# Capped attention and two feed-forward layers on one core: early products moved, the slots' banks joined two slots sooner, the last store halved

## What is computed

```
q, k, v: (2, 12, 448, 64); cap = 30
scores = cap * tanh(q @ k.T / sqrt(64) / cap)
attn   = exp(scores - max(scores));  attn /= sum(attn) + 1e-9
x      = (attn @ v) as (896, 768)
h = x @ w_in (768, 2048);   g = where(h > 0, h, exp(min(h, 0)) - 1);  x = g @ w_out
h = x @ w_in2;              g = max(0.01 h, h);                        y = g @ w_out2
```

## Time and profile before

| | us |
|---|---|
| median of 3 runs | 569.2 |
| lowest and highest | 568.25 and 569.87 |
| the profiled execution's own time | 569.0 |
| its span, first to last instruction | 567.2 |
| TensorE's granted clock | 1.00 of full speed, throughout |

### The profile page before, as it was taken

How to read it: one execution, slowest core, us unless ns; L and a number is a source line. 1 busy time by engine, 2 the same in 40 slices (tenths; PEclk the granted TensorE clock), 3 DMA queues, 4 the chain that set the end, 5 groups by cost and what they waited for, 6 DMA issues and landing times.

```text
span 567.2 us, 8613 instructions
## 1 busy us (share of the span) xinstructions
PE 555.2 (98%) x2908; PEld 500.5 (88%) x2908; DVE 469.7 (83%) x760; ACT 350.3 (62%) x603; POOL 285.7 (50%) x277
## 2 busy tenths in 40 slices
PE   6999999999999999999999999999999999999997
PEld 5777789899998999999999999999999998999996
DVE  5899998998785134898989999989999789999871
ACT  6999998989995445654644455536454445544440
POOL 6779999699966655552000008967576520000000
PEclk9999999999999999999999999999999999999999
DMA  5466655645333233335644422031123226436241
GB/s 173 105 157 150 148 150 134 153 114 140 95 88 76 83 112 111 112 110 166 210 135 159 139 87 82 1 112 57 58 63 103 62 80 226 143 110 218 85 173 50
DMA packets 34172, 67.07 MB, mean 118 GB/s; under 512 B 6864, under 2 KB 18768, under 8 KB 34128
## 3 DMA queue, kind: packets, MB, share of 16 engines
q1 hardware_dynamic: 33984, 66.28, 39.6%
q10 hardware_dynamic: 144, 0.23, 0.1%
HBM read 63.70 MB, written 2.80 MB: 117 GB/s over the span
## 4 chain that ended last, share of the span: by engine, by line
PE 92%; DVE 4%; ACT 2%; issue 1%; DMA 1%; ACTq 0%
PE mlp_ps L1170 9%; PE mlp_ps L1171 9%; PE mlp_ps L1172 9%; PE o_ps L1170 7%; PE o_ps L1171 7%; PE o_ps L1172 7%; PE scores L1170 5%; PE scores L1171 5%; PE scores L1172 5%; PE probs_t L1144 4%; PE probs_t L1170 4%; PE probs_t L1172 4%; PE probs_t L1171 4%; PE scores L1129 3%; PE scores L1130 3%; PE o_ps L1163 2%
## 5 line engine op out<-in xcount | busy, mean ns | idle before, releaser
L564 POOL TENSOR_TENSOR w_lo<-w_raw,w_hi 128x768 fp32r<-128x768 f32 (+1 forms) x62 | 103.2, 1666 | 55.8 <-ACT w_hi L654 51.8
L654 ACT ACTIVATE w_hi<-s_sum 128x768 fp32r<-128x768 f32 (+1 forms) x64 | 43.7, 684 | 81.1 <-DVE s_sum L919 55.2
L654 ACT ACTIVATE w_hi<-w_raw 128x768 fp32r<-128x768 f32 (+1 forms) x74 | 54.1, 733 | 31.6 <-PE o_ps L1172 16.0
L634 ACT ACTIVATE soft<-soft,neg_max 112x448 f32<-112x448 f32 x96 | 64.1, 683 | 0.5 <-DVE soft L794 0.5
L794 DVE TENSOR_SCALAR_CACHE_REDUCE soft<-soft,neg_abs 112x448 f32<-112x448 f32 x96 | 60.7, 669 | 1.8 <-ACT soft L624 1.5
L564 POOL TENSOR_TENSOR w_lo<-s_sum,w_hi 128x384 fp32r<-128x384 f32 x32 | 42.2, 1331 | 23.0 <-ACT w_hi L654 23.0
L1170 PE MATMUL mlp_ps<-x_hi,w_hi 128*128 128x448 f32 x132 | 49.2, 373 | 0.0
L624 ACT ACTIVATE soft<-scores 112x896 f32<-112x896 f32 x47 | 44.0, 937 | 7.2 <-PE scores L1130 7.2
L1172 PE MATMUL mlp_ps<-x_hi,w_lo 128*128 128x448 f32 x132 | 48.2, 365 | 0.0
L1171 PE MATMUL mlp_ps<-x_lo,w_hi 128*128 128x448 f32 x132 | 48.2, 365 | 0.0
L801 DVE TENSOR_TENSOR p_lo<-probs_t,p_hi 112x896 fp32r<-112x896 f32 x37 | 40.3, 1090 | 9.5 <-ACT p_hi L643 9.3
(11 more groups left out here) (241 smaller groups left out, 1765.3 us busy)
## 6 DMA issues: line engine op xcount, KB each, us to landing
w_raw<-w_units SPq DMA_DIRECT2D x120, 384.0 KB, 3.1
q_raw<-qT SPq DMA_DIRECT2D x24, 224.0 KB, 3.1
k_raw<-kT SPq DMA_DIRECT2D x23, 224.0 KB, 2.8
v_raw<-v_rows SPq DMA_DIRECT2D x24, 112.0 KB, 3.6
inv_all<-inv_rows SPq DMA_DIRECT2D x24, 112.0 KB, 3.1
y_t<-y_out SPq DMA_DIRECT2D x12, 224.0 KB, 2.8
inv_rows<-row_inv SPq DMA_DIRECT2D x24, 1.8 KB, 2.6
k_raw<-kT ACTq DMA_DIRECT2D x1, 224.0 KB, 3.1
```

The costliest lines, as they stand in the source:

```text
L564: pool.tensor_tensor(w_part(w_lo, n), w_source(n), f32(w_part(w_hi, n)), ALU.subtract).then_inc(w_lo_pool, 1)
L634: nc.scalar.activation(soft[0:QT, b, t, :], soft[0:QT, b, t, :], ACT.Exp, bias=neg_max[:, c, t:t + 1], scale=-1.0, accum_out=row_sum[:, h ...
L654: nc.scalar.activation(w_part(w_hi, n), w_source(n), ACT.Copy).then_inc(w_hi_done, 1)
```

## The change

Five things are changed.

- `EARLY` begins in step 22. Steps 22 to 30 now hold 2, 1, 3, 1, 3, 1, 1, 0 and 3 chunks (before 0, 0, 3, 1, 3, 1, 3, 1 and 3). Step 22 has chunks 0 and 1 of unit 0; step 24 has chunks 2 and 3 of unit 0 and chunk 1 of unit 1.
- To have the banks for it, `ALONE_P` goes from 22 to 20 and `TWO_BANKS` from 10 to 8, and units take banks 5, 6, 7 in turn. Slot 21 goes through `probs_t`, and slots 21 and on wait for the `p_low` of the slot just before. Heads 9 and 10 use the first bank of `o_ps` and wait for the head before. Unit 0 waits for head 7 to be read, units 1 and 2 for the `p_low` of slot 19.
- The cast and split of unit 3's weights move from steps 26 and 27 to steps 28 and 29. Unit 3's first two chunks move from step 33 to the end of step 32. In step 33 `p_high` and `p_low` of slot 31 come ahead of the activation of unit 1, and `p_low` also ahead of the maxima of slot 33.
- One chunk moves from step 49 to step 48.
- The last add is done in two halves of 224 columns; SP stores the first half and ACT the second.

```diff
-ALONE_P = 22
+ALONE_P = 20
-TWO_BANKS = 10
-EARLY = {24: ((0, (0, 1, 2)),), 25: ((0, (3,)),), 26: ((1, (0, 1, 2)),), ...
+TWO_BANKS = 8
+EARLY = {22: ((0, (0, 1)),), 23: ((1, (0,)),), 24: ((0, (2, 3)), (1, (1,))), ...
+PARTS_FIRST = 33
-MIXED = {31: (0, 0, 1), 32: (0, 1, 0), 33: (0, 2, 0), ... 48: (2, 1, 0), 49: (1, 2, 0), ...
+MIXED = {31: (0, 0, 1), 32: (0, 1, 2), 33: (0, 0, 0), ... 48: (2, 2, 0), 49: (1, 1, 0), ...
...
         def unit_bank(u):
-            return bank((6, 7, 5)[u % MLP_BANKS])
+            return bank((5, 6, 7)[u % MLP_BANKS])
...
+        def halves_of_last(t):
+
+            return [slice(0, SEQ)] if t < HC - 1 else [slice(0, SEQ // 2), slice(SEQ // 2, SEQ)]
...
@@ SyncE, the output stores @@
-                    sp.dma_start(out[rows_half * HC + t, :, batch * SEQ:(batch + 1) * SEQ], y_out[:, HC * i + t, :]
-                                 ).then_inc(y_stored, 16)
+                    cols = slice(0, SEQ) if i < 3 else halves_of_last(t)[0]
+                    sp.dma_start(out[rows_half * HC + t, :, batch * SEQ + cols.start:batch * SEQ + cols.stop],
+                                 y_out[:, HC * i + t, cols]).then_inc(y_stored, 16)
...
@@ GpSimd @@
-                if s == 27:
+                if s == 29:
                     split_w(AHEAD)
...
@@ ScalarE @@
+                if s == PARTS_FIRST:
+                    p_high(s - 2)
                 for u in units_ending_at(s - 1):
                     hidden(u)
-                if 2 <= s <= SLOTS + 1:
+                if 2 <= s <= SLOTS + 1 and s != PARTS_FIRST:
                     p_high(s - 2)
-                if s == 26:
+                if s == 28:
                     w_high(AHEAD)
...
+            cols = halves_of_last(HC - 1)[1]
+            act.wait_ge(y21_done, 2 * HC + 1)
+            act.dma_start(out[2 * HC - 1, :, cols], y_out[:, 4 * HC - 1, cols]).then_inc(y_last, 16)
+            act.wait_ge(y_last, 16)
...
@@ VectorE @@
             for s in range(STEPS):
+                if s == PARTS_FIRST:
+                    p_low(s - 2)
                 if s < SLOTS:
                     maxima(s)
                 for u in units_ending_at(s - 1):
                     hidden(u)
-                if 2 <= s <= SLOTS + 1:
+                if 2 <= s <= SLOTS + 1 and s != PARTS_FIRST:
                     p_low(s - 2)
...
-                nc.vector.tensor_tensor(y_out[:, 3 * HC + t, :], kept_u2[1][:, t, :], banks_of[1]["p4"][t], ALU.add
-                                        ).then_inc(y21_done, 1)
+                for cols in halves_of_last(t):
+                    nc.vector.tensor_tensor(y_out[:, 3 * HC + t, cols], kept_u2[1][:, t, cols], banks_of[1]["p4"][t][:, cols],
+                                            ALU.add).then_inc(y21_done, 1)
...
@@ TensorE, hidden @@
-                if u < 2:
+                if u == 0:
+                    pe.wait_ge(o_read, TWO_BANKS)
+                elif u < MLP_BANKS:
                     pe.wait_ge(p_lo_done, ALONE_P)
-                elif u == 2:
-                    pe.wait_ge(o_read, TWO_BANKS)
```

More of the change, by code:

```diff
@@ L39 @@
 BIG = 3.0e38
-ALONE_P = 22
+ALONE_P = 20
 DIRECT = 8
-TWO_BANKS = 10
-EARLY = {24: ((0, (0, 1, 2)),), 25: ((0, (3,)),), 26: ((1, (0, 1, 2)),), 27: ((1, (3,)),), 28: ((2, (0, 1, 2)),),
-         29: ((2, (3,)),), 30: ((0, (4,)), (1, (4,)), (2, (4,)))}
+TWO_BANKS = 8
+EARLY = {22: ((0, (0, 1)),), 23: ((1, (0,)),), 24: ((0, (2, 3)), (1, (1,))), 25: ((1, (2,)),), 26: ((1, (3,)), (2, (0, 1))),
+         27: ((2, (2,)),), 28: ((2, (3,)),), 30: ((0, (4,)), (1, (4,)), (2, (4,)))}
 FIRST_LOADS = (7, 11, 15, 19, 23, 26, 29)
 STEPS = 55
+PARTS_FIRST = 33
 MLP_BANKS = 3
-MIXED = {31: (0, 0, 1), 32: (0, 1, 0), 33: (0, 2, 0), **{s: (2, 2, 0) for s in range(34, 48, 2)},
-         **{s: (1, 1, 0) for s in range(35, 48, 2)}, 48: (2, 1, 0), 49: (1, 2, 0), 50: (2, 1, 0), 51: (2, 0, 4),
+MIXED = {31: (0, 0, 1), 32: (0, 1, 2), 33: (0, 0, 0), **{s: (2, 2, 0) for s in range(34, 48, 2)},
+         **{s: (1, 1, 0) for s in range(35, 48, 2)}, 48: (2, 2, 0), 49: (1, 1, 0), 50: (2, 1, 0), 51: (2, 0, 4),
          52: (0, 0, 6), 53: (0, 0, 6), 54: (0, 0, 8)}
@@ L299, in build @@
         w_loaded = [sem(f"w_loaded{i}") for i in range(RAW)]
-        y_stored = sem("y_stored")
+        y_stored, y_last = sem("y_stored"), sem("y_last")
         zero_set, ident_set, ident_ready = sem("zero_set"), sem("ident_set"), sem("ident_ready")
```

## The result

| | before | after |
|---|---|---|
| median of 20 runs each, us | 568.27 | 569.50 |
| lowest of them | 567.99 | 568.94 |
| the profiled execution's own time | 569.0 | 569.27 |
| its span | 567.2 | 567.5 |

The ratio of after to before is 1.0020, with a 95% interval of 1.0013 to 1.0027: the change costs 1.1 us (0.7 to 1.5), less than the 0.3% that the prediction calls no change. 570.2 us was forecast, with a range of 567.3 to 571.4; the forecast difference was +0.98. The forecast time started from 569.2, the median of three runs of the kernel before; the median of twenty is 568.27, so 570.2 lies 0.7 too high, and the difference is what to compare. The range holds the time of before as well, so that the time fell into it says little; the rows say more.

A forecast was written before the change was run, and what follows sets the result against it. PE was taken to set the time, losing it only in waits on one slot's chain or x_lo. Terms summed to +0.98 us, from 569.0 to 570.0 profiled, 570.2 as median; own range 569.4 to 571.0, 8-in-10 range 567.3 to 571.4.

The forecast's parts named there:

- Steps 22 to 24: Early matmuls and shared banks: waits of 0.84 for slot 20's p_lo and 1.0 for POOL's x_lo; +0.44 us.
- Steps 28 and 29: Nine matmuls fewer, but slot chain of 3.15 and ACT's cast leave them only 0.42 us shorter; +1.41 us.
- Steps 32 and 33: Two chunks of unit 3 fill step 32's wait, and their 6 matmuls leave step 33; -1.22 us.
- steps 33 and 34: DVE's full queue delays slot 32's p_lo, so step 35 starts 8.34 us after step 33; +1.1 us.
- Steps 48 and 49: Three matmuls moved from step 49 fill step 48's wait for p_lo; -0.55 us.
- The last store: Last add and store in halves: shorter landing against dearer adds, between -0.36 and +0.3; taken as -0.2 us.
- B: Rival, chance 0.16: chunk 3 and slot 32 don't wait, DVE and POOL having more give; 568.1 us.
- C: Rival, chance 0.16: as B, and steps 28 to 30 lose nothing because the chain is shorter; 566.7 us.
- D: Rival, chance 0.17: DVE's queue stays the limit after step 35, 0.3 us each in four steps; 571.4 us.
- E: Rival, chance 0.04: step 22's products find unit 0's bank or weights not ready and run in step 23; 570.4 us.

The follow-up runs named there:

- e1: Changed kernel with chunk 3 of unit 0 moved from step 24 to 25 and chunk 2 of unit 1 from 25 to 24; ratio to kernel before 1.0003.
- e11: Changed kernel with slots 20 and 21 on their own bank pairs, chunk 3 of unit 0 left in step 24; ratio to kernel before 1.0035.
- e6: Kernel before with only the changed kernel's banks, no matmul moved; ratio to kernel before 1.0042.
- e7: Changed kernel with ALONE_P at 22, chunks of steps 22 to 30 spread otherwise, unit 3's cast back in step 26; ratio to kernel before 0.9984.
- e5: Changed kernel with the cast and split of unit 3's weights back in steps 26 and 27; ratio to kernel before 1.0009.
- e4: Changed kernel with steps 31 to 33 as before, including the old order of p_hi and p_lo; ratio to kernel before 1.0024.
- e8: e7 with two more chunks in step 33, later chunks two places sooner, p_hi and p_lo in their old place; ratio to kernel before 0.9989.
- e2: Kernel before with only one chunk moved from step 49 to step 48; ratio to kernel before 0.9992.
- e3: Kernel before with only the last add and store in two halves, the second issued by ACT; ratio to kernel before 1.0002.
- e12: e8 with two more chunks in step 47, one more in step 50, two in step 51 ahead of the products, none behind; ratio to kernel before 0.9971.
- e10: e8 with one more chunk in step 50, one fewer in 51, and slot 45's p_hi and p_lo first in step 47; ratio to kernel before 0.9987.

## Why the prediction was right

Its sum was +0.98; measured were +1.0 by the profiled executions' parts and +1.1 by the ratio of the runs. So near a hit is in part luck: one term had the wrong reason and nearly the right size, and the small misses of the others cancel. Term by term, in the order of the prediction:

- **Steps 22 to 24, +0.44.** Step 23's transposes stand 3.67 after step 22's (72.97 - 69.30 = 3.67 forecast), step 25's 81.57 - 69.64 = 11.93 after them (11.91 forecast), and the wait ahead of chunk 3 is 0.9 (1.0 forecast), with the named releaser. Before, it was 9.64, with 9 matmuls less: +0.46. e1 and e11 show that the second wait is real and set by POOL alone. The wait ahead of step 23's transposes is the forecast 0.84 (69.64 + 2.83 = 72.47 against 73.31). But as the price of the shared banks, "what it costs by the rows", it is too low: by e6 they cost 0.99 over the stretch and 1.32 in steps 22 and 23, and 0.84 is what is left when six early matmuls lie under the wait. The price that the prediction put at nothing, that of one bank for heads 8 and 9, is nothing in after only because PE comes late to step 23: without the gate (e7, e11) it waits about 0.6 there.
- **Steps 28 and 29, +1.41.** Step 28 took 3.16 (3.15 forecast), both 6.91 (6.80): +1.52. The size held, the reason did not. "The cast itself was hidden in step 26 and costs 0.45 here" failed: e5 takes it out and gains nothing. The step used ACT's round of 3.65 and 0.96 from p_hi to p_lo; DVE's own round of 3.75 is as long, ends 0.1 later and doesn't contain the cast. The earlier trace rows show only its first p_lo, though the trace of before had the second at 95.68, and the two numbers were nearly the same by chance.
- **Steps 32 and 33, -1.22, and steps 33 and 34, +1.1.** Step 32 lasts 3.46 with 13 matmuls and without wait; step 35 starts 118.45 - 110.23 = 8.22 after step 33 (8.34 forecast), released by p_lo, whose round on DVE is 117.22 - 112.15 = 5.07 (5.19 before). Net -0.24 by e4 in these steps where -0.12 was forecast. The queue on DVE was full, as the prediction took it: 5.07 without a gap. What it didn't ask is whether step 33 had to be emptied, and the order changed for it: e8 has the same chunks in step 32 and ACT's and DVE's old order, fills step 33 and doesn't wait in steps 33 and 34 (step 35 lasts 0.15 more than its content).
- **Steps 48 and 49, -0.55.** Step 48 lasts 3.21 without wait; e2 alone gives -0.60.
- **The last store, -0.2.** 3.24 against 3.37, and 3.23 in e3: -0.13. The two adds of half the width take 0.38 each (0.69 for both in the row), so 0.07 of what the shorter landing gives is lost there. Both halves land 1.7 after their issue, 1.9 to 2.0 before for the whole. The Trainium skill (DMA: Bandwidth & Descriptors, Issuing engines are not separate DMA queues) says that DMAs issued from several engines share the same 16 DMA engines and that this saves only the time to issue. No run here shows it: none issues both halves from SP, so what the second engine gives and what half the bytes give are not told apart.

Of the rivals, B and C fall with step 24's wait. D falls too: from step 35 to step 47 of after the transposes stand 4.02 to 4.44 apart, the content of 16 and 18 matmuls. E falls too: the early products are in step 22. On the banks the prediction set the Trainium skill's rule (Perfetto Trace Analysis, Optimizing Tensor Performance, Matmuls) beside a cost of 0.84; the trace of e6 agrees with the rule and gives 0.99 for the stretch.

## What to carry to other kernels

A wait for another engine is worth what work you can put into it: e12 won 1.8 us by filling waits, while e10, which put the awaited instruction first, moved the wait one step on and made it larger. Find the round that is full on each engine (start of one p_lo to start of the next, with no gap between the rows) before naming the instruction that costs; here ACT's and DVE's were equal within 0.1, and taking the cast's 0.83 off ACT gave nothing. When matmuls are moved, count them by the side of the wait on which they stand, not by step.
